# Attention and two feed-forward layers: the raw buffers of the early attention items are packed, and the first two late items are loaded together

## The reference

```python
scores = 0.125 * q @ k.T            # masked where the query's block of 64 lies before the key's
attn = exp(scores - max) / (sum + 1e-9)
x = attn @ v                        # to (2304, 512)
h = x @ moe_w_in                    # 512 -> 2048
g = where(h >= 1, h, where(h <= -1, 0, (h + 1)**2 / 4))
x = g @ moe_w_out                   # 2048 -> 512
h = x @ moe2_w_in
out = (h * cos(h)) @ moe2_w_out
```

## Time and profile before

| | us |
|---|---|
| median of 3 runs | 1034.27 |
| the runs | 1034.9, 1034.27, 1034.19 |
| the profiled execution's own time | 1034.9 |
| its span in the profile | 1033.1 |

### The profile page before, as it was taken

How to read it: one execution, slowest core, us unless ns; L and a number is a source line. 1 busy time by engine, 2 the same in 40 slices (tenths; PEclk the granted TensorE clock), 3 DMA queues, 4 the chain that set the end, 5 groups by cost and what they waited for, 6 DMA issues and landing times.

```text
span 1033.1 us, 19545 instructions
## 1 busy us (share of the span) xinstructions
PE 982.7 (95%) x7296; PEld 931.1 (90%) x7296; DVE 682.2 (66%) x1613; ACT 582.8 (56%) x1232; POOL 416.5 (40%) x446
## 2 busy tenths in 40 slices
PE   5688999999999999999999999999999999999998
PEld 4588999999998999999999999899999999999996
DVE  5667777877777777777742279665565665656564
ACT  5677767666665666666632356545444544445443
POOL 4458766555464564655532222222222222222221
PEclk9699999999999999999999999999999999999999
DMA  5234322311212212221110045010100101011000
GB/s 168 94 108 157 97 91 83 104 52 56 93 53 63 86 56 74 73 77 52 63 32 22 27 158 184 1 41 0 41 21 20 41 0 41 0 41 41 0 21 21
DMA packets 30886, 63.31 MB, mean 61 GB/s; under 512 B 3680, under 2 KB 11872, under 8 KB 30816
## 3 DMA queue, kind: packets, MB, share of 16 engines
q1 hardware_dynamic: 29664, 58.21, 18.2%
q10 hardware_dynamic: 1152, 4.19, 1.0%
HBM read 52.95 MB, written 9.44 MB: 60 GB/s over the span
## 4 chain that ended last, share of the span: by engine, by line
PE 75%; DVE 12%; ACT 7%; issue 4%; DMA 1%; POOL 0%; ACTq 0%; POOLq 0%; DVEq 0%
PE hidden L1235 32%; PE acc L1254 18%; PE acc L1268 12%; PE heads_out L1158 5%; PE scores L1111 4%; PE turned L1127 2%; DVE q_parts L852 1%; DVE pt_lo L906 1%; ACT probs L680 1%; DVE stats L871 1%; DVE wout_lo L954 1%; DVE work L974 1%; DVE x_lo L968 1%; PE hidden L1202 1%; PE heads_out L1127 1%
## 5 line engine op out<-in xcount | busy, mean ns | idle before, releaser
L609 POOL TENSOR_TENSOR g_lo<-work,g_hi 128x512 fp32r<-128x512 f32 x144 | 187.5, 1302 | 433.6 <-ACT g_hi L777 433.4
L1235 PE MATMUL hidden<-x_hi,win_hi 128*128 128x256 f32 x1128 | 318.9, 283 | 1.1 <-DVE work L979 1.1
L1235 PE MATMUL hidden<-x_hi,win_lo 128*128 128x256 f32 x1128 | 314.3, 279 | 3.1 <-POOL v_parts L585 1.8
L1235 PE MATMUL hidden<-x_lo,win_hi 128*128 128x256 f32 x1128 | 313.1, 278 | 0.0
L1235 PEld LDWEIGHTS hidden<-x_hi,win_hi 128*128 128x128 f32 x1128 | 212.4, 188 | 4.9 <-DVE work L979 1.3
L1235 PEld LDWEIGHTS hidden<-x_hi,win_lo 128*128 128x128 f32 x1128 | 212.3, 188 | 5.0 <-POOL v_parts L585 2.4
L1235 PEld LDWEIGHTS hidden<-x_lo,win_hi 128*128 128x128 f32 x1128 | 212.7, 189 | 3.6
L1268 PE MATMUL acc<-g_hi,wout_lo 128*128 128x256 f32 x576 | 162.0, 281 | 9.8 <-DVE pt_lo L906 8.4
L1268 PE MATMUL acc<-g_hi,wout_hi 128*128 128x256 f32 x576 | 166.7, 289 | 0.4 <-ACT y_stage L760 0.4
L1268 PE MATMUL acc<-g_lo,wout_hi 128*128 128x256 f32 x576 | 160.1, 278 | 0.0
L579 POOL TENSOR_SCALAR probs<-probs,stats 128x320 f32<-128x320 f32 (+2 forms) x160 | 98.1, 616 | 145.1 <-DVE stats L901 144.3
(11 more groups left out here) (118 smaller groups left out, 1907.2 us busy)
## 6 DMA issues: line engine op xcount, KB each, us to landing
qk_raw<-qk_late SPq DMA_DIRECT2D x32, 480.0 KB, 3.5
qk_raw<-qk_early SPq DMA_DIRECT2D x32, 256.0 KB, 2.7
v_raw<-v_late SPq DMA_DIRECT2D x32, 160.0 KB, 3.5
x_raw<-x_scratch SPq DMA_DIRECT2D x9, 512.0 KB, 3.8
out<-y_stage SPq DMA_DIRECT2D x36, 128.0 KB, 2.4
x_raw<-w_in SPq DMA_DIRECT2D x8, 512.0 KB, 3.7
y_stage<-w_out SPq DMA_DIRECT2D x8, 512.0 KB, 3.5
x_scratch<-y_stage ACTq DMA_DIRECT2D x8, 512.0 KB, 2.9
```

The lines of the kernel that those rows point to most:

```text
L609: nc.gpsimd.tensor_tensor(g_lo[:, m % G_RING, :], work[:, m % 2, :], g_hi[:, m % G_RING, :], ALU.subtract).then_inc(g_lo_made, 1)
L1235: last = nc.tensor.matmul(into, w[:, p, c, half * P:(half + 1) * P], x[:, c, :], start=(i == 0), stop=(i == len(products) - 1))
```

## The change

Early items use raw buffers of their own size: the even half starts at column 0 as before, the odd half at column 512 of `qk_raw` instead of 960, and at column 128 of `v_raw` instead of 320. The first late item's 960 columns then overlap both early halves, so its load may no longer be issued when item 30 is split, but only when item 31 is. SP now issues the loads of items 32 and 33 together behind the split of item 31, and the v loads of 32 and 33 together behind the split of item 31's v.

```diff
         def raw_qk(n):
-            at = (n % 2) * QKV_COLS[1]
+            at = (n % 2) * QKV_COLS[late(n)]
             return qk_raw[:, at:at + QKV_COLS[late(n)]]
...
         def raw_v(n):
-            at = (n % 2) * 5 * D
+            at = (n % 2) * chunks_of(n) * D
             return v_raw[:, at:at + chunks_of(n) * D]
...
+            def same_kind_of_raw(n):
+
+                return n < ITEMS and n not in (HEADS, HEADS + 1)
+
             def after_split(n):
 
                 sp.wait_ge(q_lo_made, n + 1)
                 sp.wait_ge(k_lo_made, n + 1)
-                if n + 2 < ITEMS:
+                if same_kind_of_raw(n + 2):
                     load_qk(n + 2)
+                if n == HEADS - 1:
+                    load_qk(HEADS)
+                    load_qk(HEADS + 1)
 
             def after_split_v(n):
                 sp.wait_ge(v_lo_made, n + 1)
-                if n + 2 < ITEMS:
+                if same_kind_of_raw(n + 2):
                     load_v(n + 2)
+                if n == HEADS - 1:
+                    load_v(HEADS)
+                    load_v(HEADS + 1)
```

## The result

| | before | after |
|---|---|---|
| median, us | 1034.51 (6 runs, 1033.38 to 1035.15) | 1040.03 (6 runs, 1037.18 to 1042.36) |
| profiled execution, its own time | 1034.9 | 1041.69 |
| its span | 1033.1 | 1039.9 |

The changed kernel is slower: ratio 1.0054, 95% interval 1.0044 to 1.0064, which is 5.5 us on the medians (4.6 to 6.6). The forecast was 1036.9 with a range to 1038.8. The sign is right; the size is not: the forecast lies 2.4 us above this median of before, and 5.5 us came.

A forecast was written before the change was run, and what follows sets the result against it. PE, busy for 95% of the span, was taken as the bound. Its standstill of 2.6 us, with clock, v loads and addresses at nothing, on the median 1034.27 gave 1036.9 us, 0.25% slower; range 1035.0 to 1038.8.

The forecast's parts named there:

- Where the loads are issued, and the chain to PE: Pair issued at 177.87 and about 178.24; ACT's k_hi of item 32 4.33 us late, PE stands still 2.6 us.
- When it lands: Item 32's q and k load takes 4.4 us, lengthened by a code packet, and lands at 182.27.
- Rival B: At item 32's load, the second load slows the first by up to 1.7 us: 1037.7 us; chance 0.08.
- The clock: Behind PE's standstill the forecast has the clock stay at 1.00, so it adds nothing.
- rival C: PE's clock falls after the standstill, losing 1.7 us more, 4.3 in all: 1038.6 us; chance 0.13.
- I count nothing more here: Behind the standstill every engine is late by the same amount, 2.6 to 2.7 us, with no further cost.
- The v loads, the addresses: Item 32's v load has 2.0 us of cover and costs nothing; the moved odd early half is taken as 0.
- Rival D: PE's pt_lo waits, 8.4 us between 200 and 520 us, shrink and give the delay back: 1034.3 us; chance 0.12.

The follow-up runs named there:

- swapped: Changed kernel with item 33's q and k load issued first and item 32's behind it; 1041.65 us, ratio 1.0060.
- changed, again: The changed kernel timed and profiled once more with no edit, also called the repeat; 1040.2 us, ratio 1.0046.
- longer standstill: Changed kernel with item 33's q and k load first and item 32's issued only when that one has landed; 1043.95 us, ratio 1.0090.
- the control: Kernel before with 64 increments of an unused semaphore at the start of PE's program; 1041.23 us, ratio 1.0069.
- addresses only: Kernel before with early items packed, the load order kept and qk_raw 64 columns longer; 1034.45 us, ratio 0.9990.
- both earlier splits: Changed kernel with item 31's four split steps moved ahead by 4 slots (1037.52 us, ratio 1.0019) or 6 slots (1036.46 us, ratio 1.0011).

## Why the prediction was wrong, step by step

- **Where the loads are issued, and the chain to PE: right.** The pair is issued at the moment named, ACT waits for it, and the arithmetic of the cover holds: ACT's start is 184.84 - 2.08 - 177.94 = 4.82 late, less 1.65 of idle time and 0.10 of slack on PE makes 3.07, and 3.05 were measured. That PE stood one matmul earlier, for POOL's v part, and not at `weigh` for `pt_lo`, changed nothing in the sum: that matmul was 2.68 us late and `weigh`, which then waited for `pt_lo`, 3.00, so the chain that I had followed is the one that ended last. I had read the two PE rows and not the wait that PE's program places ahead of them.
- **When it lands: the reason right, the size short.** I took 4.4 us from the row of the same moment, with the code packet as its cause. The packet hit the load in all five profiles of kernels that kept PE's code and the issue time, and shifting the code removed it. But the load took 4.7 to 5.3, not 4.4 (in "swapped" the pair's first load, item 33's there, took 4.2). One row was too little to read the size from: at this moment a 480 KB load with the packet in it and no second one right behind it took 4.1 to 4.9 us (five profiles: 4.1, 4.4, 4.4, 4.7, 4.9), and the first of a pair 4.2 to 5.3 (four profiles). Without the packet it was 3.1 to 3.4 alone and 3.6 to 3.9 as the first of a pair. So the packet is worth 1.1 to 1.2 us and the second load 0.4 to 0.5, as differences of the means. Rival B's full sharing (1.7 us) is excluded, and its 1.7 us of transfer was too much as well: the second load lands 1.2 us behind the first. The Trainium skill, DMA: Bandwidth & Descriptors, section Queues, rings and completion order, has each DMA engine take the descriptors of one queue in the order of the ring; from that I had worked out that the second transfer adds nothing. The traces agree with the order and not quite with the nothing: the load ahead comes later by some tenths. This error is worth 0.5 to 0.9 us.
- **The clock: this is the step that failed.** The forecast put the clock's part at nothing. I gave rival C, a fall behind the standstill for 1.7 us, 0.13, because 2.6 us lay between a stretch with a fall and a wait of 1.9 without one. The clock fell behind the standstill in four of the five profiles with 2.4 to 3.1 us, and in none of the three with 0.75 to 1.47 us. Where it fell, the place cost 1.5 us more than the standstill explains (changed, again: ACT starts 181.74 + 1.47 - 177.94 = 5.27 us late, less the cover of 1.75 is 3.5, and 5.06 were measured; longer standstill: 186.90 - 1.70 - 177.94 - 1.75 = 5.5, and 7.01 were measured). My 1.7 for a fall was about right, its chance was not. And the forecast's own standstill was underestimated in the direction that makes a fall likelier. The length of the standstill isn't all that decides, though: 2.39 us were followed by a fall and 2.53 were not. What also differs between the profiles is when the standstill comes after the clock's last rise. In three profiles with the last rise at 83 to 86 us, the standstill of 2.53 us began 97.3 us after it and those of 2.39 and 3.07 us began 98.5 us after it. No run changed the one without the other, so the moment stands beside the length as an untested cause.
- **"I count nothing more here" was wrong as well.** The wait near 323 us, 140 us behind the place, has nearly the same length in all kernels (1.81 to 1.90 us), yet the clock fell behind it in all six profiles with a standstill of 2.4 us or more and in one of the seven others (the six rows of that kind in the table and the control). Each such fall is 1.5 us. That the two go together is a count over thirteen profiles. The traces narrow down how: the lengths of this wait with and without a fall overlap, so its length doesn't decide, and what differs is how long after the clock's last rise it begins. In the five profiles with a fall at the place, the rise that ends this fall lies 136.6 to 137.9 us ahead of the wait, whether the standstill was 2.4 or 5.0 us long, and the next fall begins 139.95 us behind the rise in every one of them. These are two such stretches of the repeat, in the columns of the earlier trace rows:

```profile
187.50:327.40 139.90, 134.00 (x1081) 130.84 (x1081) 108.79 (x332) 89.41 (x206) 76.33 (x81) 1.00 0.22 69
327.50:330.80 3.30, 3.30 (x14) 3.12 (x13) 2.19 (x7) 1.04 (x3) 0.61 (x2) 0.50 0.50 184
```

In the other eight the last rise lies in the opening. There the wait was followed by a fall at 236.8 ("addresses only") and 240.0 us (changed) after it, and by none at 238.0 to 238.1 (before and both earlier splits), 260.9, 265.2 and 265.4 us. So a fall at the place seems to bring the second one about by setting the moment, and not by the delay. No run was made to test this, so the cause stays open.
- **The v loads, the addresses: right.** Each alone leaves the time where it was.
- **Rival D**, that the delay is given back, did not happen: PE's waits for `pt_lo` sum to the same behind the place (the nine of the earlier trace rows).

```profile
PE acc L1278 <- DVE pt_lo L916: 8.3, 9, 1.8
```

Put together, and as an estimate, since only profiled executions show their parts: the 5.5 us of the medians are about 3.0 to 3.5 us of standstill, 1.5 us in a part of the executions for the fall behind it, and 1.5 us in more executions than before for the fall near 328 us. The sum of these for an execution with both is 6.0 to 6.5. How many executions of the changed kernel have each fall isn't known; one of its two profiles has the first, and both have the second. The opening's clock spreads the runs of both kernels by a further 1 to 2 us either way and belongs to neither.

No version beat both kernels. Packing the early items costs nothing where `qk_raw` has 64 more columns, as "addresses only" shows.

## What to carry to other kernels

When a layout makes a load wait for one more reader, compare the moment at which the last reader ends with the moment at which the data is first wanted: here they were 0.07 us apart, so a whole load's time was exposed, less the 1.75 us of cover behind it. Price PE's standstill together with its clock: here, up to 1.5 us of standstill cost only itself, and 2.4 us and more cost 1.5 us on top in five of six profiles. Of a load that is waited for, look at the load at that very moment and at what else runs on the queues, and give it a range: one row read 4.4 us, and such loads took 4.1 to 5.3. When a step is moved ahead of others to issue a load earlier, price what it delays on its own engine: DVE's moved q split cost 1.3 us where 0.4 had been expected.

## What the runs showed of the hardware

- A code packet (16 KB) that runs among a 480 KB load's packets can make the load 1.1 to 1.2 us longer: 4.1 to 4.9 us with no second load right behind it against 3.1 to 3.4 at the same place without it. Near the load's end it cost nothing (3.2 us in the control). Whether it hits changed with 64 instructions at the very start of PE's program: the packet stayed near 179 to 180 us while the load's issue came 4.3 us later, and a wait 180 us into the kernel got more than 1 us shorter.
- Two 480 KB loads issued 0.38 us apart on one queue landed 1.2 us apart in all seven profiles that have the pair, and the first took 0.4 to 0.5 us longer than one without a second load right behind it.
- 64 semaphore increments in PE's program, where it was waiting anyway until 5.1 us, delayed its first matmul by 5.84 us, so one takes at least 0.09 us.
- In the longest standstill the clock fell while PE was still idle, and the loss behind it was the same 1.5 us as where it fell afterwards.
